# Convolution-mixing and two MLPs on one core: 128-row matmuls replaced by two alternating streams of 64-row matmuls

## What is computed

```python
w = np.exp(weight_gen - np.max(weight_gen, axis=-1, keepdims=True))
w = w / (np.sum(w, axis=-1, keepdims=True) + 1e-09)
out = np.einsum('bshk,bskhg->bshg', w, x_unf)       # x_unf: the last 7 rows of x

h = x @ w_in                                        # moe: 192 -> 2048
g = np.maximum(0.01 * h, h)
x = g @ w_out                                       # 2048 -> 192

h = x @ w_in                                        # moe2, with its own weights
g = np.where(h > 0.0, h, np.exp(np.minimum(h, 0.0)) - 1.0)
return g @ w_out
```

## Time and profile before

| | |
|---|---|
| median of 3 runs | 1212.63 us (1212.58 to 1213.23) |
| the profiled execution | 1211.23 us, of it 1209.4 us span |
| TensorE busy | 1185.8 us (98%), 5208 matmuls |
| DVE busy | 814.8 us (67%) |
| ACT busy | 746.2 us (62%) |
| GpSimd busy | 355.1 us (29%) |
| DMA | 54.24 MB, mean 45 GB/s |

### The profile page before, as it was taken

One profiled execution on the slowest core, in us unless ns is written; L12 is line 12 of the kernel. 1 busy time (PEld: TensorE's weight loads), 2 busy tenths in 40 slices (PEclk: granted clock), 3 DMA queues, 4 the chain that ended last, 5 costly groups with the idle time before them and its releaser, 6 DMA issues.

```text
span 1209.4 us, 14562 instructions
## 1 busy us (share of the span) xinstructions
PE 1185.8 (98%) x5208; PEld 973.0 (80%) x5208; DVE 814.8 (67%) x778; ACT 746.2 (62%) x815; POOL 355.1 (29%) x216
## 2 busy tenths in 40 slices
PE   7798999999999999999999999999999999999998
PEld 5586888888888888888888888888888888888887
DVE  7877775766767666675766767666676766766555
ACT  3365757666575665757666575665756656575675
POOL 5725060240704206061250704307061250700000
PEclk9999999999999999999999999999999999999999
DMA  7231112011110211112010110211112010100001
GB/s 194 61 98 37 27 40 64 26 49 26 51 51 26 66 35 49 26 39 62 26 49 26 47 54 26 63 39 49 26 39 62 26 49 26 39 26 27 14 17 36
DMA packets 44642, 54.24 MB, mean 45 GB/s; under 512 B 4116, under 2 KB 32914, under 8 KB 44624
## 3 DMA queue, kind: packets, MB, share of 16 engines
q1 hardware_dynamic: 44624, 54.01, 14.7%
HBM read 36.29 MB, written 17.69 MB: 45 GB/s over the span
## 4 chain that ended last, share of the span: by engine, by line
PE 92%; DVE 5%; ACT 1%; DMA 0%; POOL 0%; issue 0%; SPq 0%; POOLq 0%; ACTq 0%
PE hidden L516 46%; PE y_b L545 9%; PE y_b L546 9%; PE y_a L552 9%; PE y_a L551 9%; PE y_a L550 9%; DVE hid_lo L952 1%; DVE hidden L913 1%; ACT hid_hi L810 1%; DVE up_b_lo L832 1%; DVE up_a_lo L832 1%; DMA xw<-in_x_dram 0%; PE turn L585 0%; DVE dn L345 0%; PE turn L589 0%; DVE dn L344 0%
## 5 line engine op out<-in xcount | busy, mean ns | idle before, releaser
L952 DVE TENSOR_TENSOR hid_lo<-hidden,hid_hi 128x1024 fp32r<-128x1024 f32 x254 | 311.0, 1225 | 242.0 <-ACT hid_hi L810 242.0
L810 ACT ACTIVATE hid_hi<-hidden 128x1024 fp32r<-128x1024 f32 x254 | 260.8, 1027 | 329.3 <-DVE hidden L913 200.8
L284 POOL TENSOR_TENSOR mix<-xw,wk 128x768 f32<-128x768 f32 x15 | 23.3, 1554 | 684.8 <-DVE wk L859 681.8
L916 DVE SCALAR_TENSOR_TENSOR hidden<-act,hidden 128x1024 f32<-128x1024 f32 x129 | 157.5, 1221 | 98.7 <-ACT act L785 96.7
L516 PE MATMUL hidden<-in_a_hi,up_a_hi 128*128 128x512 f32 x510 | 200.8, 394 | 12.2 <-DVE hid_lo L952 11.6
L545 PE MATMUL y_b<-hid_hi,dn 128*128 128x512 f32 x512 | 199.5, 390 | 1.2 <-DVE dn L345 1.2
L546 PE MATMUL y_b<-hid_lo,dn 128*128 128x512 f32 x512 | 199.3, 389 | 0.0
L552 PE MATMUL y_a<-hid_lo,dn 128*128 128x512 f32 x512 | 199.2, 389 | 0.0
L550 PE MATMUL y_a<-hid_hi,dn 128*128 128x512 f32 x512 | 199.2, 389 | 0.0
L551 PE MATMUL y_a<-hid_hi,dn 128*128 128x512 f32 x512 | 199.2, 389 | 0.0
L516 PE MATMUL hidden<-in_b,up_b_lo 128*128 128x512 f32 x510 | 199.0, 390 | 0.0
(11 more groups left out here) (100 smaller groups left out, 1140.9 us busy)
## 6 DMA issues: line engine op xcount, KB each, us to landing
xw<-in_x_dram SPq DMA_DIRECT2D x14, 960.0 KB
raw_b<-squares_out SPq DMA_DIRECT2D x60, 96.0 KB, 2.2
out_dram<-staged SPq DMA_DIRECT2D x15, 384.0 KB, 2.4
squares_in<-prod SPq DMA_DIRECT2D x56, 96.0 KB, 2.0
squares_out<-ya SPq DMA_DIRECT2D x15, 256.0 KB, 2.0
raw_a<-squares_in SPq DMA_DIRECT2D x14, 256.0 KB, 2.8
raw_d<-in_moe_w_out_dram SPq DMA_DIRECT2D x8, 384.0 KB, 6.2
raw_a<-in_moe_w_in_dram SPq DMA_DIRECT2D x8, 256.0 KB, 4.9
```

The costliest lines, as they stand in the source:

```text
L284: ops.tensor_tensor(dst, src, w, ALU.mult).then_inc(done, 1)
L810: nc.scalar.activation(hid_hi[:, s % 2, :], hidden[:, s % 2, :], ACT.Copy).then_inc(s_hi, 1)
L916: nc.vector.scalar_tensor_tensor(out=h, in0=a, scalar=-1.0, in1=h, op0=ALU.add, op1=ALU.max).then_inc(done, 1)
L952: nc.vector.tensor_tensor(hid_lo[:, s % 2, :], h, hid_hi[:, s % 2, :].bitcast(f32), ALU.subtract).then_inc(s_lo, 1)
```

## The change

**Pairs of 64-row matmuls.** Each 128-row matmul becomes two, of rows 0 to 63 (LOW) and 64 to 127 (HIGH). They are issued alternately, and the two of a pair always write different PSUM banks: in `up` the LOW one writes one half of `hidden` and the HIGH one the other; in `down` `y_a` has a bank for each (`y_a[0]`, `y_a[1]`), and `y_b` is written by LOW beside a HIGH `y_a`, later by HIGH beside a LOW `y_a`. The product with `up_b_lo`, which used both halves of the rows with the 64 features, is now needed for 64 rows alone per half, so both halves of the hidden features share one pair (`up_pair`); for this the high part of the 64 features also stands in rows 64 to 127 of a new `in_b_up`, and `up_b_lo` has half as many columns. A step is then 19 pairs instead of 20 matmuls.

```diff
-            def up(m, src, g, s):
-                for i in (0, 1):
...
+            def up(m, src, g, s, second):
...
+                if not second:
+                    for n in range(3):
+                        up_a(LOW, 0, n)
+                        up_a(HIGH, 1, n)
+                    up_b(LOW, 0)
+                    up_b(HIGH, 1)
+                    up_pair(m, src, s)[1].then_inc(s_open, 1)
+                    return
+
+                pe.wait_ge(s_open, g)
+                for n in range(3):
+                    up_a(LOW, 1, n)
+                    up_a(HIGH, 0, n)
+                half1 = up_b(LOW, 1, stop=True)
+                half0 = up_b(HIGH, 0, stop=True)
```

```diff
                     if not (known(ph) and ph == 0 and s < 2):
 
-                        pe.wait_ge(s_lo, g - 1)
-                    up(m, input_of(m, c), g, s)
+                        pe.wait_ge(s_g if (dm if s < 2 else m) else s_lo, g - 1)
+                    up(m, input_of(m, c), g, s, False)
...
+                    pe.wait_ge(s_lo, g - 1)
+                    of, step = (dm, ST - 2 + s) if s < 2 else (m, s - 2)
+                    down_open(of, step, g - 2, ph if s == 2 and dm is not None else None)
+                    if s == 1:
+
+                        down_close(of, step, g - 2)
+                        up(m, input_of(m, c), g, s, True)
+                    else:
+                        up(m, input_of(m, c), g, s, True)
+                        down_close(of, step, g - 2)
```

```diff
-                        act_e.wait_ge(s_g, g - 1)
+                        act_e.wait_ge(s_lo, g - 1)
...
-                    nc.vector.scalar_tensor_tensor(out=h, in0=a, scalar=-1.0, in1=h, op0=ALU.add, op1=ALU.max).then_inc(done, 1)
+                    nc.vector.scalar_tensor_tensor(out=a, in0=a, scalar=-1.0, in1=h, op0=ALU.add, op1=ALU.max).then_inc(done, 1)
...
-                    nc.vector.tensor_tensor(hid_lo[:, s % 2, :], h, hid_hi[:, s % 2, :].bitcast(f32), ALU.subtract).then_inc(s_lo, 1)
+                    nc.vector.tensor_tensor(hid_lo[:, s % 2, :], (act if m else hidden)[:, s % 2, :], hid_hi[:, s % 2, :].bitcast(f32), ALU.subtract).then_inc(s_lo, 1)
```

```diff
+                    if s == 1 and dm is not None:
+                        take_y(dm, dc, ph - 1)
                     act_e.wait_ge(s_up, g + 1)
...
-                    if s == 1 and dm is not None:
-                        take_y(dm, dc, ph - 1)
...
+                dve.wait_ge(s_ya1, ph + 1)
+                a0, a1 = y_a[0][:, :], ya[dm][:, :]
...
+                nc.vector.tensor_tensor(a1, a0, a1, ALU.add).then_inc(s_ya, 1)
```

More of the change, by code:

```diff
@@ L521, in up_first, with up_pair @@
+            def up_pair(m, src, s, stop=False):
+                cols = slice(s * P, (s + 1) * P)
+                low = nc.tensor.matmul(hidden[:, s % 2, HALF[0]], up_b_lo[m][LOW, cols], in_b[src][LOW, :], start=False, stop=stop)
+                high = nc.tensor.matmul(hidden[:, s % 2, HALF[1]], up_b_lo[m][HIGH, cols], in_b_up[src][HIGH, :], start=False, stop=stop)
+                return low, high
             def up_first():
@@ L548, in down_a @@
-            def down_a(m, f, hi, lo):
-                nc.tensor.matmul(y_a[:, :], dn[m][:, f, 0:P], hi, start=(f == 0), stop=False)
-                nc.tensor.matmul(y_a[:, :], dn[m][:, f, 2 * P:3 * P], hi, start=False, stop=False)
-                return nc.tensor.matmul(y_a[:, :], dn[m][:, f, 0:P], lo, start=False, stop=(f == FT - 1))
-            def down(m, s):
-                for i in (0, 1):
-                    hi, lo = hid_hi[:, s % 2, HALF[i]], hid_lo[:, s % 2, HALF[i]]
-                    down_b(m, 2 * s + i, hi, lo)
-                    last = down_a(m, 2 * s + i, hi, lo)
-                last.then_inc(s_dn, 1)
+                low, high = up_pair(0, input_of(0, 0), 0, stop=True)
@@ new lines, in up_first, with down_b, down_a @@
+                low.then_inc(s_up1, 1)
+                high.then_inc(s_up, 1)
+            def down_b(m, s, rows, i, n):
+                f = 2 * s + i
+                v = (hid_hi, hid_lo)[n]
+                start, stop = f == 0 and n == 0 and rows == LOW, f == FT - 1 and n == 1 and rows == HIGH
+                return nc.tensor.matmul(y_b[:, :], dn[m][rows, f, P:2 * P], v[rows, s % 2, HALF[i]], start=start, stop=stop)
+            def down_a(m, s, rows, i, n):
+                f = 2 * s + i
+                first, v = ((0, hid_hi), (2 * P, hid_hi), (0, hid_lo))[n]
+                bank = y_a[0] if rows == LOW else y_a[1]
+                return nc.tensor.matmul(bank[:, :], dn[m][rows, f, first:first + P], v[rows, s % 2, HALF[i]],
+                                        start=(f == 0 and n == 0), stop=(f == FT - 1 and n == 2))
@@ L584, in sum_first_mix @@
                     for j in range(J):
-                        last = nc.tensor.matmul(turn_cols[:, 0, j], term[:, j, 0:P], ident[:, :], start=False, stop=(end and j == J - 1))
+                        last = nc.tensor.matmul(by_token(turn_a)[:, j], term[:, j, 0:P], ident[:, :], start=False, stop=(end and j == J - 1))
                     if end:
@@ L696, in mlp1_input_hi @@
                 else:
+                    nc.scalar.activation(in_b_up[n][D2:P, :], b, ACT.Copy)
                     nc.scalar.activation(in_b[n][0:D2, :], b, ACT.Copy).then_inc(s_xhi, 1)
@@ L809, in phase @@
                         act_e.wait_ge(s_dn, g - 1)
-                    nc.scalar.activation(hid_hi[:, s % 2, :], hidden[:, s % 2, :], ACT.Copy).then_inc(s_hi, 1)
+                    nc.scalar.activation(hid_hi[:, s % 2, :], (act if m else hidden)[:, s % 2, :], ACT.Copy).then_inc(s_hi, 1)
             softmax_exp(0)
```

224 lines of the change are left out of this document (145 added, 79 removed).

## The result

The changed kernel takes **1242.07 us** (median of 4 runs, 1242.01 to 1243.4), the kernel before 1212.76 in the same comparison: ratio 1.0243, 95% interval 1.0228 to 1.0259, slower by 2.4%. Predicted were 1235 us, 1204 to 1264, slower with 0.73.

A forecast was written before the change was run, and what follows sets the result against it. TensorE, busy throughout 120 to 1180 us, was taken as the bound. New waits of 5.3 us against 3.6 saved per pair of phases gave 21 us; with start +1, last phases -0.6, end +1.2: 1235 us, range 1204 to 1264.

The forecast's parts named there:

- Price of a pair: Time on TensorE of two half-row matmuls side by side, taken as 227 ns, the beat of a full matmul.
- 0.30: Rival: the second half's weight load comes too late, a pair takes 0.30 us, 1475 us in all; chance 0.06.
- 240 ns: Rival: each half-row matmul pays its own 13 ns, so a pair takes 240 ns, 1262 us in all; chance 0.13.
- no overlap: Rival: the two half-row streams don't overlap, 38 beats or 8.6 us a step, 2160 us in all; chance 0.04.
- 213 ns: Rival: the 13 ns beyond the bare columns vanish, about 1222 us; pairs of 213 to 227 ns together had 0.57.
- B: Start of a leaky phase: TensorE waits for the input's low half in_b, late by 1.84 us.
- C: Leaky step 3: its first pair overwrites step 1's PSUM buffer and waits for its release, late by 0.94 us.
- D: Leaky steps 6 and 7: step 7 waits for DVE, behind two slow subtractions, late by 1.48 us.
- E: ELU step 3: down of step 1 is allowed 5.67 us and needs 6.57, late by 0.90 us.
- F: Other ELU steps: ACT is 0.44 us late, then TensorE goes by the loop, 4.35 for 4.31; 0.1 us in all.
- The start: First phases, where TensorE waits for a DVE that also splits weights: saved beats worth nothing there, +1 us.
- the chains keep up: Rival: predicted waits stay away and TensorE remains the bound, 1161 us (1201 with half the waits); chance 0.20 for both.

The follow-up runs named there:

- e2: Changed kernel with the second part of up two down pairs behind the first (none in step 2), copies and additions of y behind step 1's activation: 1202.45 us.
- e4: Changed kernel with e2's edits, both input halves split in ELU step 5, DVE's slow subtractions in leaky steps 3 and 5, transpose back in step 6: 1184.36 us.
- e7: Kernel before, full-row matmuls in the old order, one product left out in one half, so 19 per step (part of the computation missing): 1163.60 us.
- e5: Changed kernel with the first matrix's up_b_lo split by one 128 by 512 DVE op per quarter instead of two of 64 by 256: 1240.24 us.
- e12: Changed kernel with the second matrix's up_b_lo split by one DVE op per quarter instead of two: 1238.20 us.
- e10: Changed kernel with only the copies and additions of y moved behind step 1's activation, TensorE's order kept: 1323.68 us.
- e8: Changed kernel with the leaky layer's activation written to SBUF (act) like the ELU layer's, instead of staying in PSUM: 1264.33 us.

## Why the prediction was right, and where it was off

**Direction and cause held.** The saved beats were outweighed by new waits of TensorE, 1.61 us per pair of phases where 1.6 were predicted; the run is 7 us above the forecast, at the upper end, 1242, of the forecast's own range. e2 to e4 show the cause, not only the place: the same pairs without these waits are faster than the kernel before. The phases came as stated too: from the first `up` of a leaky phase (674.30), its wait ahead of it included, to that of the ELU phase (711.09) it is 38.5 us, and the ELU phase takes 35.8 (38.5 and 35.4 predicted). Of the places named for waits, leaky step 6 had almost none, 0.11 us.

**Price of a pair: right**, 0.227 us, but not by the reason given. I had let two loads follow each other at 0.11 us and just fit under the beat. They start together, so they would have left room. In the rule that stood beside it, from the Trainium skill, "TensorE: Matmul & The Clock Gate", section "LDWEIGHTS (loading the stationary operand)", a load costs by its columns and not by its rows. With that the trace agrees: a load of 64 rows reads 0.18 us, one of 128 rows 0.19. The estimate of 213 ns drawn from it put two loads one behind the other, and the rows show them side by side. The rivals of 0.30 (with the estimate of 0.295 beside it), 240 ns, no overlap and 213 ns are all excluded by the rows at 702.5, 0.46 us for two pairs.

**The waits, one by one.** I count each from the start of the `up` or `down` group ahead of it to the group behind it, less its beats, since the first pair after a wait also loses 0.11 to 0.15 us (its row reads 0.50 for 0.39); a beat is 226.7 ns here:

| | predicted | measured |
|---|---|---|
| B, start of a leaky phase | 1.84 | 2.00 |
| C, leaky step 3 | 0.94 | 0.99 |
| D, leaky step 7 | 1.48 | 1.09 |
| E, ELU step 3 | 0.90 | 0.73 |
| F and all else | 0.1 | 0.56 |
| sum | 5.3 | 5.37 |

D was too large, and one of its two subtractions did get shorter: the group of `in_a_lo` went from 1858 to 1432 ns (`in_b` from 1762 to 1736).

```profile
L997 DVE TENSOR_TENSOR in_b<-yb,in_b 64x512 fp32r<-64x512 f32 x16 | 27.8, 1736 | 0.5
L995 DVE TENSOR_TENSOR in_a_lo<-ya,in_a_hi 128x512 fp32r<-128x512 f32 x16 | 22.9, 1432 | 0.0
```

F was too small: many groups start 0.02 to 0.1 us late, leaky step 6 loses 0.11, and the first `down` of ELU step 2, which waits for y, 0.22. That the sum fits to 0.1 is partly the luck of errors of both signs. And a steady pair of the kernel before was already 0.13 us over its 320 beats (72.67 to 72.54), so 5.24 of the 5.37 are new; less the 3.63 saved that is the 1.61.

**The ELU loop: right**, 4.35 us from one relu to the next, on ACT in the order of time:

```profile
733.31 1.01 ACT L893 ACTIVATE act<-hidden 128x1024 f32<-128x1024 f32 x1
734.34 1.06 ACT L895 ACTIVATE act<-act 128x1024 f32<-128x1024 f32 x1
736.69 1.06 ACT L918 ACTIVATE hid_hi<-act 128x1024 fp32r<-128x1024 f32 x1 [1.29 <-DVE act L1040]
737.66 1.01 ACT L893 ACTIVATE act<-hidden 128x1024 f32<-128x1024 f32 x1
```

`hid_lo` stayed at 1.23 us with both sources in SBUF, where GpSimd does not mix.

**The start was mis-sized: +1 predicted, +8.5 measured**, the one term that failed. "Beats saved ahead of such a wait are worth nothing" was nearly right: in e7, with 19 beats in the old order, the first three phases take 146.0 us instead of 148.1, 2.1 us for some 5.4 us of beats. But the same bound, a DVE that also splits the weights, meant that what the change adds to that splitting counts, and I costed the two 64-row ops, which take the place of one, at nothing. They are 1.4 us longer at 33 and at 89 us, beside GpSimd, and 5.5 us longer over all eight quarters; e5 and e12 together gave 4.0 us back. The other 4.5 stay open, with the lower clock of the changed kernel's start as one candidate.

**Last three phases**: -0.6 predicted, +0.2 measured. **End**: +1.2 predicted, +1.1 measured. Behind the last matmul, where the earlier trace rows had one copy, stand ACT's copy, DVE's two additions and then the transpose:

```profile
1233.46 0.59 ACT L825 ACTIVATE ylow<-y_b 64x512 f32<-64x512 f32 x1 [0.37 <-PE y_b L587]
...
1234.09 0.68 DVE L1011 TENSOR_TENSOR yb<-y_b,ylow 64x512 f32<-64x512 f32 x1 [2.94 <-ACT ylow L825]
1234.70 0.67 DVE L1017 TENSOR_TENSOR ya<-y_a_rows,ya 128x512 f32<-128x512 f32 x1
...
1235.43 0.33 PE L703 MATMUL hidden<-ident,ya 128*128 128x128 f32 x1 [2.00 <-DVE ya L1017]
```

**The rival "the chains keep up"** (1161) did not occur, but e7 gives 1163.60 where the order is left alone. Its number was right for another kernel: the chains can keep up with 19 beats, and it is the new order that stops them.

## What to carry to other kernels

A busy share of 98% on one engine says nothing of how far the others are behind it: read the loop time of the others and the time from a result to its use, in beats, before taking beats away. Where a saving comes with a new order of issue, cost each consumer's allowed time in that order; here the order cost more than the saving gave, and moving half of `up` three pairs forward, with the copies that hang on it, turned 2.4% slower into 0.8% faster. Work added to an engine that is the bound in the start counts for most of its time, though it is done only once (4.0 of 5.5 us here). And a wait can cost more than its length: in e10 the granted clock fell behind many of them.

## What was not expected of the hardware

- Weight loads for the two halves of the rows run at the same time: both start at 702.52 and read 0.18 us, as one does. With them and the matmuls side by side, a pair of 64-row matmuls of 512 columns costs one beat of 0.227 us, as one of 128 rows does.
- ACT's copy of 1024 columns takes 1061 ns from SBUF and 1027 ns from PSUM.
- Beside GpSimd, a DVE subtraction of 64 rows by 256 columns that reads SBUF twice takes 1.7 us (two in 3.45), one of 128 rows by 512 columns 2.03 us; without it the two take 0.84 together and the one 0.68. Narrow pieces lose most there.
- The same contention makes `hid_lo` of 1024 columns mostly 1.6 to 2.2 us, at most 2.71, for 1.22 (e8), but only where both sources are in SBUF; with one in PSUM it stays at 1.22 beside GpSimd.
- In e10 the granted clock fell to 0.50, 1.2 GHz, within 1 us of a wait of 2.97 us, and pairs of 64-row matmuls then came 0.43 us apart.
